# Chunked attention before a feed-forward chain: 32 queries against their own 64 keys, without masks

## The reference

```python
for c in range(nc):                      # chunk, left_ctx, right_ctx = 32, 16, 8
    l_start = max(0, c * 32 - 16)
    r_end = min(S, c * 32 + 32 + 8)
    k_full = np.concatenate([mem_k, k[:, :, l_start:r_end]], axis=2)
    v_full = np.concatenate([mem_v, v[:, :, l_start:r_end]], axis=2)
    scores = scale * np.matmul(q[:, :, c*32:c*32+32], k_full.transpose(0, 1, 3, 2))
    scores = scores - np.max(scores, axis=-1, keepdims=True)
    a = np.exp(scores)
    a = a / (np.sum(a, axis=-1, keepdims=True) + 1e-09)
    out[:, :, c*32:c*32+32] = np.matmul(a, v_full)
x = elu(x @ w_in) @ w_out                # first layer, x is the attention's output
out = (s * relu(x @ w_in2)**2 + b) @ w_out2
```

## Time and profile before

| | |
|---|---|
| median of 3 runs | 1122.68 us (1121.28 to 1123.22) |
| profiled execution | 1121.61 us, span 1119.7 us |
| TensorE busy | 1090.9 us, 97% |
| VectorE, ScalarE, GpSimd busy | 830.9, 790.0, 343.4 us |
| mean granted TensorE clock | 0.996 |
| moved by DMA | 273.44 MB, 244 GB/s |

### The profile page before, as it was taken

How to read it: one execution, slowest core, us unless ns; L and a number is a source line. 1 busy time by engine, 2 the same in 40 slices (tenths; PEclk the granted TensorE clock), 3 DMA queues, 4 the chain that set the end, 5 groups by cost and what they waited for, 6 DMA issues and landing times.

```text
span 1119.7 us, 18242 instructions
## 1 busy us (share of the span) xinstructions
PE 1090.9 (97%) x5787; PEld 871.0 (78%) x5787; DVE 830.9 (74%) x1240; ACT 790.0 (71%) x1866; POOL 343.4 (31%) x373
## 2 busy tenths in 40 slices
PE   8999999999999999999999999999999999999998
PEld 5777677766777777787887887888888888888886
DVE  5895798479977746988968968869657578566485
ACT  4997877786777657668768677587676476774574
POOL 5343787577123333104465032761000000000000
PEclk9999999999999999999999999999999999999999
DMA  9966868778798998979899698997696666776664
GB/s 196 199 123 205 259 177 262 221 222 257 205 281 246 263 266 242 311 238 390 282 356 339 194 334 308 356 336 243 204 308 198 189 193 199 217 216 190 194 198 152
DMA packets 195990, 273.44 MB, mean 244 GB/s; under 512 B 111928, under 2 KB 120120, under 8 KB 195896
## 3 DMA queue, kind: packets, MB, share of 16 engines
q1 hardware_dynamic: 195896, 272.28, 78.5%
HBM read 196.74 MB, written 75.50 MB: 243 GB/s over the span
## 4 chain that ended last, share of the span: by engine, by line
PE 80%; ACT 6%; DVE 6%; issue 4%; DMA 2%; POOL 1%; SPq 0%; ACTq 0%; DVEq 0%; POOLq 0%
PE ps L1099 37%; PE ps L1084 32%; PE ps L990 3%; ACT ps L1184 2%; PE ps L984 1%; DMA w_ring<-w_scratch 1%; ACT elu L1277 1%; PE ps L1015 1%; PE ps L999 1%; PE ps L951 1%; DVE g_lo L1603 1%; DVE att L1448 1%; PE ps L972 1%; ACT elu L1282 1%; PE ps L1042 1%
## 5 line engine op out<-in xcount | busy, mean ns | idle before, releaser
L1084 PE MATMUL ps<-xc_hi,w_ring 128*128 128x512 f32 x1248 | 400.1, 394 | 2.8 <-ACT s L1250 1.0
L1099 PE MATMUL ps<-g_hi,w_ring 128*128 128x512 f32 x1248 | 389.5, 393 | 8.3 <-DVE g_lo L1603 3.4
L1099 PEld LDWEIGHTS ps<-g_hi,w_ring 128*128 128x128 f32 x1248 | 232.1, 189 | 61.4 <-issue 4.4
L1084 PEld LDWEIGHTS ps<-xc_hi,w_ring 128*128 128x128 f32 x1248 | 234.3, 188 | 56.0 <-ACT s L1250 1.5
L1099 PE MATMUL ps<-g_lo,w_ring 128*128 128x512 f32 x624 | 243.9, 391 | 0.0
L1084 PE MATMUL ps<-xc_lo,w_ring 128*128 128x512 f32 x624 | 243.0, 389 | 0.0
L1603 DVE TENSOR_TENSOR g_lo<-X,g_hi 128x512 fp32r<-128x512 f32 x240 | 178.2, 748 | 22.5 <-ACT g_hi L1317 21.9
L1317 ACT ACTIVATE g_hi<-X 128x512 fp32r<-128x512 f32 x240 | 150.3, 630 | 59.2 <-PE ps L1099 55.2
L849 POOL TENSOR_TENSOR w_raw<-w_raw 128x256 fp32r<-128x256 f32 x100 | 99.4, 999 | 260.6 <-ACT w_raw L1335 260.6
L1517 DVE TENSOR_TENSOR X<-s,ps 128x512 f32<-128x512 f32 x96 | 65.6, 684 | 105.3 <-ACT s L1250 92.2
L1099 PEld LDWEIGHTS ps<-g_lo,w_ring 128*128 128x128 f32 x624 | 117.4, 188 | 24.9
(11 more groups left out here) (165 smaller groups left out, 1528.5 us busy)
## 6 DMA issues: line engine op xcount, KB each, us to landing
w_ring<-w_scratch SPq DMA_DIRECT2D x280, 512.0 KB, 4.4
w_scratch<-w_raw SPq DMA_DIRECT2D x100, 256.0 KB, 5.4
w_scratch<-w_ring SPq DMA_DIRECT2D x64, 256.0 KB, 3.3
w_raw<-in_moe_w_in SPq DMA_DIRECT2D x16, 512.0 KB, 5.1
w_raw<-in_moe_w_out SPq DMA_DIRECT2D x16, 512.0 KB, 6.3
w_scratch<-w_later SPq DMA_DIRECT2D x24, 256.0 KB, 3.0
x_scratch<-y SPq DMA_DIRECT2D x12, 512.0 KB, 5.8
att<-x_scratch SPq DMA_DIRECT2D x12, 512.0 KB, 6.3
```

Source lines behind the costliest of these rows:

```text
L1084: last = nc.tensor.matmul(bank_of(st, st.i), w[:, a, cols], x[:, st.pi, kk, :], start=(st.pi in (P1, P5) and kk == 0 and n == 0), stop=(kk ...
L1099: last = nc.tensor.matmul(bank_of(st, d), w[:, a, cols], x[:, k % RING, :], start=(st.pi in (P1, P5) + (P4,) * (1 - st.gr) and st.i == 0 a ...
```

## The change

A query's products are cut to its own chunk. The 96 queries of a unit stay together; within it each chunk's 32 queries meet only their 64 keys (8 of memory, 56 of context). KEYS is 64 now.

- copy_kT (VectorE) writes windows: for each chunk 8 memory columns (copied only when a batch begins) and 56 columns of context, which overlap between chunks. It is on VectorE before and after; in the woven part it moves to another step.
- score: 24 products of 64 x 32 against 64 x 64; a mask product (1 x 32 against 1 x 64 for four heads) is left only for the first chunk and the last chunk of a batch. chunk_of and may_see go.
- maximum and exponentials: VectorE takes the maximum and subtracts it into E (SBUF); ScalarE has one exponential over 96 x 512 in place; VectorE sums E, takes the reciprocal and multiplies into P.
- transpose_p: 4 transposes of 128 columns, one bank; copy_PT all on ScalarE.
- V lies in windows as well: keys of heads 0 to 3 of a window at partitions 0 to 63, of heads 4 to 7 at 64 to 127. A unit's v comes in 6 transfers (3 chunks, two halves of the heads), with memory rows by further ones when a batch begins. In the head it is loaded 4 units ahead (V_AHEAD).
- p_times_v: 24 products of 64 x 64 against 64 x 32.
- score in the head waits for sub_done (the subtraction) instead of P_ready, and so do the first steps of the layer.
- Woven: each unit begins two steps later; K_T is three steps ahead of Q_T (after P_T of the unit before); transpose_q waits for place_x of unit n-2 and score for that of n-1.
- The zero fills ahead of the loads, and the waits for them, go; two blocks at a batch's edge take a small load in their place.

```diff
-KEYS = CTX + MEM
+WIN = LEFT + CHUNK + RIGHT
+KEYS = MEM + WIN
+V_AHEAD = 4
-WOVEN = [(HEAD + c, 10 + 12 * c) for c in range(UNITS - HEAD)]
-K_T, Q_T, SC, MAX, EXP_E, EXP_O, NORM, P_T, PV = 0, 1, 3, 4, 5, 6, 7, 10, 12
+WOVEN = [(HEAD + c, 12 + 12 * c) for c in range(UNITS - HEAD)]
+K_T, Q_T, SC, MAX, EXP, NORM, P_T, PV = -3, 0, 3, 4, 5, 6, 9, 12
...
+def v_loads(n):
+    return 2 * CHUNKS + (2 if n < HEAD else 2 * CHUNKS) * new_mem_v(n) + 2 * unfilled(n, V_AHEAD)
...
             load_qk(0)
+            stage_mem_v(0)
             for n in range(AHEAD):
                 if n + 1 < AHEAD:
                     load_qk(n + 1)
-                load_v(n)
+                if n < V_AHEAD:
+                    load_v(n)
...
             def transpose_q(n):
-                if n < HEAD:
-                    pe.wait_ge(kT_sb, n + 1)
-                else:
-                    pe.wait_ge(x_placed, placed(n - 1))
+                pe.wait_ge(kT_sb, n + 1)
+                if n >= HEAD:
+                    pe.wait_ge(x_placed, placed(n - 2) if n > HEAD else placed(n - 1))
...
             def score(n):
                 if n < HEAD and n >= 2:
-                    pe.wait_ge(P_ready, n - 1)
+                    pe.wait_ge(sub_done, n - 1)
+                if n > HEAD:
+                    pe.wait_ge(x_placed, placed(n - 1))
                 pe.wait_ge(qT_sb, n + 1)
                 pe.wait_ge(kT_sb, n + 1)
...
                 for j in range(PAIRS):
-                    for e in range(2):
-                        half = slice(64 * e, 64 * e + 64)
-                        last = nc.tensor.matmul(pairs(s_bank(n) + e, QU, KEYS)[:, j, :], qT[i][half, j, :],
-                                                kT[i][half, j, :], start=False, stop=True, skip_group_check=True)
+                    s, jj = divmod(j, 2)
+                    for c in range(CHUNKS):
+                        own = slice(CHUNK * c, CHUNK * c + CHUNK)
+                        for e in range(2):
+                            half = slice(64 * e, 64 * e + 64)
+                            last = nc.tensor.matmul(S_of(n)[own, e, 2 * jj + s, :], qT[i][half, j, own], kT[i][half, j, c, :],
+                                                    start=c != at_edge, stop=True, skip_group_check=True)
...
             def p_times_v(n):
...
+                for c in range(CHUNKS):
+                    own = slice(CHUNK * c, CHUNK * c + CHUNK)
+                    for jj in range(2):
+                        for s in range(2):
+                            keys = slice(64 * s, 64 * s + 64)
+                            for e in range(2):
+                                lane = 2 * jj + e
+                                last = nc.tensor.matmul(X_banks[64 * e:64 * e + 64, s, jj, own],
+                                                        v_of(n)[keys, c, lane * D:(lane + 1) * D],
+                                                        PT_of(n)[keys, 2 * e + jj, own], start=True, stop=True,
+                                                        skip_group_check=True)
...
-            def exps(n, e):
-                i = slot_of(n)
...
+            def exps(n):
+                act.wait_ge(sub_done, n + 1)
+                e = E[slot_of(n)][:, :, 0:KEYS]
+                nc.scalar.activation(e, e, ACT.Exp).then_inc(exp_done, 1)
...
-                nc.vector.tensor_copy(kT[slot_of(n)][:, :, :], kT_bank(n)).then_inc(kT_sb, 1)
+                to, of = kT[slot_of(n)], kT_bank(n)
+                if new_mem_k(n):
+                    nc.vector.tensor_copy(to[:, :, :, 0:MEM], of[:, :, CTX:CTX + MEM].unsqueeze(2)
+                                         .to_broadcast([128, PAIRS, CHUNKS, MEM]))
+                windows = bass.AP(of.tensor, of.offset, [of.ap[0], of.ap[1], [CHUNK, CHUNKS], [1, WIN]])
+                nc.vector.tensor_copy(to[:, :, :, MEM:KEYS], windows).then_inc(kT_sb, 1)
 
             def maximum(n):
...
+                nc.vector.tensor_tensor(E[i][:, :, 0:KEYS].rearrange("p (e g) t -> p e g t", e=2), S_of(n), most,
+                                        ALU.subtract).then_inc(sub_done, 1)
```

More of the change, by code:

```diff
@@ L248, in woven_at, with new_batch, new_mem_k, new_mem_v @@
 def woven_at(g):
-    return [(n, g - w0) for n, w0 in WOVEN if 0 <= g - w0 <= PV]
+    return [(n, g - w0) for n, w0 in WOVEN if K_T <= g - w0 <= PV]
+def new_batch(n, lag):
+    return n < lag or (n - lag) // UPB != n // UPB
+def new_mem_k(n):
+    return new_batch(n, 2 if n < HEAD else 1)
+def new_mem_v(n):
+    return n == HEAD or new_batch(n, V_AHEAD if n < HEAD else 1)
+def unfilled(n, ahead):
+    return n < ahead and n % UPB in (0, UPB - 1)
+def qk_loads(n):
+    return 2 + new_mem_k(n) + unfilled(n, AHEAD)
+def v_loads(n):
+    return 2 * CHUNKS + (2 if n < HEAD else 2 * CHUNKS) * new_mem_v(n) + 2 * unfilled(n, V_AHEAD)
+def qk_count(n):
+    return 16 * sum(qk_loads(m) for m in (range(n % AHEAD, n + 1, AHEAD) if n < HEAD else range(HEAD, n + 1)))
+def v_count(n):
+    return 16 * sum(v_loads(m) for m in (range(n % V_AHEAD, n + 1, V_AHEAD) if n < HEAD else range(HEAD, n + 1)))
 def x_slot(n):
@@ L659, in load_v @@
             def load_v(n):
                 b, blk = divmod(n, UPB)
[L661 to L667 removed]
+                done = v_first[n % V_AHEAD] if n < HEAD else v_in
@@ new lines, in load_v @@
+                if n >= V_AHEAD:
+                    sp.wait_ge(pv_done, n + 1 - (V_AHEAD if n < HEAD else 1))
+                if new_mem_v(n) and n < HEAD:
+                    sp.wait_ge(v_staged[b], 32)
+                for s in range(2):
+                    if new_mem_v(n) and n < HEAD:
+                        at = slice(64 * s, 64 * s + MEM)
+                        sp.dma_start(v_of(n)[at], v_stage[b][at].unsqueeze(1).to_broadcast([MEM, CHUNKS, 4 * D])).then_inc(done, 16)
+                    if unfilled(n, V_AHEAD):
+                        sp.dma_start(by_four(v_of(n)[64 * s + MEM:64 * s + MEM + LEFT, 0]), four_heads(v, b, s, 0, LEFT)).then_inc(done, 16)
+                    for c in range(CHUNKS):
+                        at = 64 * s + MEM
+                        first = blk * QU + CHUNK * c - LEFT
+                        lo, hi = max(first, 0), min(first + WIN, S)
+                        if new_mem_v(n) and n >= HEAD:
+                            sp.dma_start(by_four(v_of(n)[64 * s:at, c]), four_heads(mem_v, b, s, 0, MEM)).then_inc(done, 16)
+                        sp.dma_start(by_four(v_of(n)[at + lo - first:at + hi - first, c]), four_heads(v, b, s, lo, hi)).then_inc(done, 16)
@@ L981, in score @@
                 i = slot_of(n)
[L982 to L991 removed]
+                at_edge = {0: 0, UPB - 1: CHUNKS - 1}.get(n % UPB)
@@ new lines, in score @@
+                if at_edge is not None:
+                    own = slice(CHUNK * at_edge, CHUNK * at_edge + CHUNK)
+                    unseen = edge[:, at_edge // 2, :].unsqueeze(1).to_broadcast([1, PAIRS, KEYS])
+                    for e in range(2):
+                        nc.tensor.matmul(S_of(n)[own, e], ones[:, :], unseen, start=True, stop=False, skip_group_check=True)
+                for j in range(PAIRS):
+                    s, jj = divmod(j, 2)
[5 more added lines that the diff above has]
+                                                    start=c != at_edge, stop=True, skip_group_check=True)
@@ L992, in score, with transpose_p @@
                 last.then_inc(scores, 1)
-            def transpose_p(n, e):
+            def transpose_p(n):
                 pe.wait_ge(P_ready, n + 1)
                 if n < HEAD and n:
-                    pe.wait_ge(PT_sb[e], n)
-                for j in range(PAIRS):
-                    last = nc.tensor.transpose(PT_bank(n, e)[:, j, :], P[slot_of(n)][:, PAIRS * e + j, :],
+                    pe.wait_ge(PT_sb, n)
+                for g in range(PAIRS):
+                    last = nc.tensor.transpose(PT_bank(n)[:, g, :], P[slot_of(n)][:, 128 * g:128 * g + 128],
```

267 lines of the change are left out of this document (120 added, 147 removed).

## The result

| | before | after |
|---|---|---|
| median | 1121.98 us (4 runs, 1120.55 to 1123.22) | 1136.72 us (4 runs, 1133.36 to 1140.24) |
| profiled execution, span | 1121.61, 1119.7 us | 1139.98, 1138.2 us |
| mean granted TensorE clock | 0.996 | 0.973 |

The ratio is 1.0132, 95% interval 1.0088 to 1.0177: the change makes the kernel slower, by 14.7 us, where 1120.1 and a range of 1112 to 1132 had been forecast.

A forecast was written before the change was run, and what follows sets the result against it. TensorE, 97% busy, was taken as the bound, with VectorE closing the head's loop alongside it. Head +4.1, woven work +3.3 and waits given back -10 sum to -2.6, so 1122.7 becomes 1120.1 us, range 1112 to 1132.

The forecast's parts named there:

- the forecast 4.1: Head: total loss in us, from periods +1.5, start +1.8 and way out +0.8.
- 3.3 - 10 = -6.7: Woven part: +3.3 us of added TensorE work and batch edges, less 10 us of waits given back.
- Product cost, 0.055 us: TensorE: each small product of scores and P times V takes 0.055 us, worked out from earlier spacings and weight loads.
- +0.21 us a unit: TensorE: net added work per unit from scores, mask, P times V and the transposes of P and k.
- The rival of 0.101: TensorE: a small product costs 0.101 us whatever its size; +70 us, about 1190; chance 0.08.
- Head's start, "so I take +1.8": Head's start: 26 more SyncE issues cost +1.8 us; from 0 if hidden to +12 if all exposed.
- SyncE's issues set the start: Head's start: k of units 2 to 5 comes late; +6 instead of +1.8, 1124.3, up to 1130; chance 0.11.
- Head's periods, 4.7: Head: TensorE's own work sets a period of 4.7 us; 13 periods with edges come to 62.1, +1.5.
- Way out, +0.8: Leaving the head for the layer: a wait goes, P times V grows, transposes shrink; +0.8 us net.
- Waits given back in the woven part, -10 of 16.4: Woven part: six tenths of 16.4 us, TensorE idle time plus clock dip, come back; bounds 0 and -16.4.
- nothing comes back: Woven part: idle time belongs to VectorE and the weights, so none returns; 1130.1; chance 0.24.
- The dip of the clock: Woven part, 152 to 155 us, after GpSimd's weights stall: 1.8 us lost; no granted clock below 1 expected afterwards.

The follow-up runs named there:

- run 4: Changed kernel with score products reordered so that four in a row use the same part of the array; 1143.6 us (1 run).
- run 10: Changed kernel, head: ScalarE issues v of heads 4 to 7 after its exponentials, SyncE the rest, one unit later at the start; 1129.8 us.
- run 6: Changed kernel with v in the head loaded only for units 0 to 3, later units using old buffer contents (output not the attention's); 1120.4 us.
- run 11: Changed kernel with ScalarE issuing half of the head's v after its exponentials, and woven q and k requested ahead of v; 1124.1 us.
- run 5: Kernel before the change, with each unit's transfer of v cut by rows into six; 1156.2 us, ratio 1.0278 to 1.0327.

## Why the prediction was wrong, step by step

The step that failed is the price of SyncE's issues in the head. The sum had 1.8 us for them at the start, and nothing in the periods and on the way out. Measured, the head lost 9.6, 6.3 and 5.9 us in these three stretches, 21.8 in place of the forecast 4.1. Behind the head the profiles differ by -3.4, where 3.3 - 10 = -6.7 had been forecast.

- **Product cost, 0.055 us: wrong, twice too high.** 0.022 for scores, 0.028 for P times V. The slope in the earlier trace rows came from products that shared the array among two halves at most; the new ones are spread over more parts of it, and run 4 shows that this is what makes them cheap. "+0.21 us a unit" was in truth -1.31, so the term for TensorE's work had the wrong sign. (It also holds a slip: the old P times V stands in it with 0.66 where the earlier trace rows give 0.63, 1 us over 32 units.) The rival of 0.101 fell with it.
- **Head's start, "so I take +1.8": here the step failed first.** It was 9.6 at unit 4 (unit 3: 31.1 instead of 24.6, 6.5). I had counted the 26 issues and the upper bound of 12 covered the truth; the reason for the low value, that issue and data overlap, did not hold, because SyncE has no pause in which to catch up (run 10, half of v on another queue, has unit 4 at 28.9). The rival "SyncE's issues set the start" had the mechanism and a chance of 0.11, but it stopped at the start: up to 1130.
- **Head's periods, 4.7: wrong in what sets them.** TensorE could have had 3.25, VectorE 4.25 (4.2 had been worked out). Measured are 62.4 / 12 = 5.2. In these 62.4 us SyncE issues for 56.9 (97 issues), before for 38.6 of 56.1 (54): each period needs 6 to 8 issues of v at 0.42 or more (0.71 for memory rows) and two or three of q and k. Without v's (run 6) the periods were 4.3 in the mean. I had asked for the queue's load only at the start; a sum over the 104 us (163 issues) would have shown a queue without slack.
- **Way out, +0.8: +5.9.** The block of v at the end of SyncE's list, a wait of 4.3 us ahead of the P times V at 109.9, and one of 2.5 us for ScalarE ahead of the fifth step. Without v's later loads (run 6) this stretch took 13.7, less than before.
- **Waits given back in the woven part, -10 of 16.4: wrong in sign.** From 112 to 440 us TensorE idles 25.5 of 328 us instead of 14.6 (18.3 to 29.0 in all other profiles of the change, but for run 4), and its mean clock is 0.97 instead of 0.99, by estimate up to 6.6 us more. Together up to 17.5; beside them the pieces save, by the head's price, 15 x 1.31 = 19.6. What is left is near the 3.4 by which this part got shorter, but the last two terms are estimates. ScalarE did lose work (211.1 busy instead of 240.3, 12% less, not the quarter forecast), but what ends TensorE's waits comes hardly sooner, so TensorE reaches it earlier and stands; run 4, with longer pieces, idles less. The longest wait shows it. Before, TensorE stood 2.5 us for GpSimd's w_ring up to 151.69. Counted from the fifth step, it now reaches this place 2.2 us earlier (47.0 instead of 49.2) and goes on 1.1 us earlier (50.5 instead of 51.7), after 3.5 us; in the chain of waits GpSimd's w_ring stands ahead of it as before. That is the rival "nothing comes back", and it took most of the gain of the pieces as well. The waits of TensorE from 112 to 360 us, as the earlier trace rows, in the changed kernel:

```profile
PE ps L1169 <- issue: 5.0, 3, 3.5
PE ps L1154 <- ACT s L1312: 4.5, 2, 3.4
PE ps L1021 <- DMA att<-in_k: 4.2, 2, 2.4
PE ps L1154 <- ACT ps L1298: 2.5, 1, 2.5
PE ps L1169 <- POOL w_early L931: 2.3, 1, 2.3
```

- **The dip of the clock: forecast to go, and it stayed.** At 152 to 155 the clock is 1.00 now, but the program is 21.8 us later there. Behind the same wait for w_ring the clock is 0.61 from 172.5 to 176.0, where it was 0.57 from 151.7 to 155.5. Windows ahead of the wait (full clock, no idle time), at the wait, and behind it:

```profile
160.00:168.00 8.00, 8.00 (x80) 6.29 (x79) 6.90 (x12) 7.28 (x16) 4.13 (x5) 1.00 0.75 188
168.50:172.50 4.00, 0.48 (x3) 0.14 (x1) 3.96 (x6) 2.02 (x6) 2.40 (x3) 0.91 0.53 199
172.50:180.00 7.50, 7.50 (x32) 5.92 (x32) 7.50 (x10) 5.76 (x14) 5.94 (x5) 0.82 0.40 149
```

- **Right:** VectorE's 4.2 a period (4.25 in run 6), the copy of k that was on VectorE already, and that ScalarE ends up with slack in the head. The upper bound of 12 for the start covered the 9.6, but the range of the whole did not cover a loss in the periods and on the way out.

Open: what makes single issues take 1 to 3 us, how the loss in the woven part divides between late loads, weights and the clock, and why the new kernels scatter so much more (1115.1 to 1129.6 in the 12 runs of run 11, against 1119.4 to 1125.5 for the 24 of the kernel before beside them).

## What to carry to other kernels

Before a load is cut into more transfers, add up what its queue issues over a whole stage, with a price for each issue from the trace, and set it against the stage's length; a queue that is at 76 of 104 us does not take 52 issues more. The price of an issue isn't fixed (in run 5 0.36 us for pieces of 20 rows, up to 2.2 for pieces of 17 to 19), so take it from the trace for the very shape. When many transfers can't be avoided, divide them over two queues, put them behind the work of the engine that issues them, and order each list by when the data is wanted. When a piece on the busiest engine gets cheaper, ask first what the others can deliver: here most of an estimated 40 us of it became waits and work at the lower clock.

## What was not expected of the hardware

- 24 products of 64 x 32 against 64 x 64 start within 0.52 us when neighbours use different parts of the array, within 1.68 when four in a row use the same.
- Half a microsecond of SyncE for a transfer of 56 KB (median 0.42 for v, 0.71 and more for the memory rows from SBUF to SBUF).
- An issue can take several times its usual price: up to 3.3 us for one of q at a DMA share of 1.08 (run 11), but also 1.7 to 2.2 us for pieces of 17 to 19 rows at a share of 0.12 (run 5), where pieces of 20 rows take 0.36. So full DMA engines aren't the only reason.
- TensorE's granted clock over the first 104 us was 0.82 in the changed kernel and 0.92 in run 4, whose fifth step came at about the same time: there TensorE was busy 90.6 us of 104 instead of 75.7.
